# A linear-attention and MoE kernel: output turned by VectorE's block transposes, key transposes parted

## The reference

```python
for t in range(S):                                   # attention with a decaying state
    state = alpha[:, :, t, :, None] * state + einsum('bhd,bhe->bhde', k[:, :, t], v[:, :, t])
    y[:, :, t] = einsum('bhd,bhde->bhe', q[:, :, t], state)
x = y as (3072 tokens, 384)
p = domain_probs / (domain_probs.sum(-1) + 1e-9)     # dense mixture, 4 experts of 1024
x = sum_e p[:, e] * (relu(x @ w1[e]) @ w2[e])
h = x @ w_in                                         # 384 -> 2048
out = (h * clip(h + 3, 0, 6) / 6) @ w_out
```

## Time and profile before

| | |
|---|---|
| median of 3 runs | 1420.34 us (1420.33 to 1421.3) |
| profiled execution | 1419.88 us, its span 1418.1 |
| busy share of the span | TensorE 98%, VectorE 52%, ScalarE 38%, POOL 59% |
| mean granted clock of TensorE | 0.996 |

### The profile page before, as it was taken

One profiled execution on the slowest core, in us unless ns is written; L12 is line 12 of the kernel. 1 busy time (PEld: TensorE's weight loads), 2 busy tenths in 40 slices (PEclk: granted clock), 3 DMA queues, 4 the chain that ended last, 5 costly groups with the idle time before them and its releaser, 6 DMA issues.

```text
span 1418.1 us, 30461 instructions
## 1 busy us (share of the span) xinstructions
PE 1388.5 (98%) x11672; PEld 1140.5 (80%) x11672; DVE 731.3 (52%) x1383; ACT 533.6 (38%) x927; POOL 837.6 (59%) x870
## 2 busy tenths in 40 slices
PE   6789999999999999999999999999999999999998
PEld 5678888888888888888888888888888888888887
DVE  6977665545554555455545455555455343333343
ACT  2133333333344333344433335433334443335553
POOL 8867776565666565656665656565655444444442
PEclk9899999999999999999999999999999999999999
DMA  4333333333333433334333333443332333233330
GB/s 142 119 120 108 102 110 96 106 93 115 93 104 124 138 93 107 93 109 128 107 115 116 93 107 93 136 123 107 93 93 82 113 118 100 90 100 92 99 123 34
DMA packets 70366, 150.10 MB, mean 106 GB/s; under 512 B 9296, under 2 KB 21840, under 8 KB 70224
## 3 DMA queue, kind: packets, MB, share of 16 engines
q1 hardware_dynamic: 70224, 148.16, 34.5%
HBM read 143.36 MB, written 4.77 MB: 104 GB/s over the span
## 4 chain that ended last, share of the span: by engine, by line
PE 93%; POOL 4%; issue 1%; DVE 1%; ACT 0%; DMA 0%; DVEq 0%; POOLq 0%; ACTq 0%
PE h_bank L446 41%; PE out_banks L462 28%; PE out_third L462 14%; PE score_banks L358 4%; POOL k_lev L828 2%; PE score_banks L420 2%; PE turn_bank L398 1%; POOL decay L802 1%; PE score_banks L414 1%; PE turn_bank L386 1%; PE turn_bank L388 1%; POOL w_lo L842 1%; PE turn_bank L374 1%; POOL k_lev L818 0%; DMA alpha_q<-qa 0%
## 5 line engine op out<-in xcount | busy, mean ns | idle before, releaser
L842 POOL TENSOR_TENSOR w_lo<-w_raw,w_hi 128x768 fp32r<-128x768 f32 x288 | 547.6, 1902 | 528.2 <-ACT w_hi L745 528.0
L739 ACT ACTIVATE h_hi<-gated 128x512 fp32r<-128x512 f32 x288 | 182.2, 633 | 670.5 <-DVE gated L590 582.3
L446 PE MATMUL h_bank<-x_hi,w_hi 128*128 128x512 f32 x864 | 336.4, 389 | 1.1 <-issue 1.1
L446 PE MATMUL h_bank<-x_lo,w_hi 128*128 128x512 f32 x864 | 336.1, 389 | 0.0
L446 PE MATMUL h_bank<-x_hi,w_lo 128*128 128x512 f32 x864 | 336.0, 389 | 0.0
L590 DVE SCALAR_TENSOR_TENSOR gated<-h_bank,probs 128x512 f32<-128x512 f32 x192 | 132.7, 691 | 328.0 <-PE h_bank L446 328.0
L604 DVE TENSOR_TENSOR h_lo<-gated,h_hi 128x512 fp32r<-128x512 f32 x288 | 241.6, 839 | 57.5 <-ACT h_hi L739 57.5
L745 ACT ACTIVATE w_hi<-w_raw 128x768 fp32r<-128x768 f32 x288 | 239.1, 830 | 8.0 <-DMA w_raw<-w 8.0
L462 PE MATMUL out_banks<-h_hi,w_hi 128*128 128x512 f32 x576 | 233.0, 405 | 0.3 <-DVE x_lo L614 0.3
L462 PE MATMUL out_banks<-h_hi,w_lo 128*128 128x512 f32 x576 | 225.0, 391 | 0.0
L462 PE MATMUL out_banks<-h_lo,w_hi 128*128 128x512 f32 x576 | 224.5, 390 | 0.0
(11 more groups left out here) (75 smaller groups left out, 1279.5 us busy)
## 6 DMA issues: line engine op xcount, KB each, us to landing
w_raw<-w SPq DMA_DIRECT2D x288, 384.0 KB, 3.1
alpha_q<-qa SPq DMA_DIRECT2D x48, 256.0 KB, 3.5
k_raw<-kk SPq DMA_DIRECT2D x48, 128.0 KB, 3.5
probs<-prob_scratch SPq DMA_DIRECT2D x6, 1024.0 KB, 7.5
v_diag<-v SPq DMA_DIRECT2D x96, 48.0 KB, 2.4
out<-result SPq DMA_DIRECT2D x18, 256.0 KB, 3.9
level_sb<-level SPq DMA_DIRECT2D x1, 80.0 KB, 3.1
ident_sb<-ident SPq DMA_DIRECT2D x1, 64.0 KB, 2.8
```

The source lines that it names most:

```text
L446: mm = pe.matmul(h_bank[g % 2][:, :], a, x, start=k == 0 and i == 0, stop=k == K3 - 1 and i == 2)
L739: act.activation(h_hi[:, g % DEEP, :], gated[:, g % 2, :], ACT.Copy).then_inc(hh_made, 1)
L842: pool.tensor_tensor(w_lo[:, g % RING, :], w_raw[:, g % RAW, :], w_hi[:, g % RING, :].bitcast(F32), ALU.subtract).then_inc(w_lo_made, 1)
```

## The change

- `attend` writes its output in another order. Weights are now 32 tokens wide instead of 64, and each matmul goes to a quarter of the partitions (`quarter(i, jp)`): eight matmuls instead of four, then sixteen instead of eight. Partitions then hold (head of the pair, pair half, 32 tokens), the free dimension (token half, 96 features).
- `copy_y` and TensorE's `turn_y` go. VectorE's new `turn_y` has two block transposes of 32x32, each of 64 partitions and 192 elements, from PSUM to `y_turned`. The rows of the first weights are ordered on the host to fit.
- `split_x` reads `y_turned`, one slot behind the state slot.
- `turn_k(n)` is parted: `turn_k(n, 0)` stays in the score visit, `turn_k(n, 1)` ends the attention visit of chunk n - 1. ScalarE copies each half for itself; the copy of half 1 stands in the slot behind the state slot. Half 0 waits for that copy. `next_state` waits for the transpose that ends its visit.
- `decay_state` moves from VectorE to ScalarE, as four activations of 48 elements, in the slot behind the score slot; in the first stage it stands ahead of `odd_k`.

The core of the diff; left out are renamed semaphores (`ys_made` is now `yt_made`), doubled counts, `TURN_AT`, buffer declarations and the order of the weight rows.

```diff
@@ -204,6 +203,10 @@
         def own(i):
             return slice(64 * i, 64 * i + 64)
+        def quarter(i, jp):
+            return slice(64 * i + 32 * jp, 64 * i + 32 * jp + 32)
         def alpha_of(n):
             return alpha_q[n % QRING][:, 0, :, :]
...
@@ -359,40 +362,22 @@
                                                start=True, stop=True)
                 mm.then_inc(p_made, 1)
-            def turn_k(n):
+            def turn_k(n, jp):
                 if n == 0:
                     pe.wait_ge(in_ident, 16)
                 pe.wait_ge(k_made, K_STEPS * (n + 1))
-                need(pe, s_made, carried(n))
-                need(pe, x_hi_made, n - 1)
-                need(pe, x_lo_made, n - 1)
-                if n % PER_TILE == 0:
-                    need(pe, x_hi_made, n)
-                    need(pe, x_lo_made, n)
-                for jp in range(2):
-                    mm = pe.transpose(kt_out[:, jp * P:(jp + 1) * P], k_level(n, LEVELS)[:, 2 * jp:2 * jp + 2, :],
-                                      ident_sb[:, :])
-                mm.then_inc(kt_made, 1)
-            def turn_y(n):
-                pe.wait_ge(ys_made, 2 * (n + 1))
-                need(pe, s_made, carried(n + 1))
-                need(pe, x_hi_made, n)
-                need(pe, x_lo_made, n)
-                rows = y_rows[n % 2]
-                for i in range(2):
-                    pe.matmul(turn_bank[own(i), P:P + CH], rows[:, P:STATE], ident_sb[:, own(i)],
-                              start=True, stop=True)
-                pe.transpose(turn_bank[:, 0:P], rows[:, 0:P], ident_sb[:, :]).then_inc(xt_made, 1)
+                if jp == 0 or n <= PER_TILE:
+                    need(pe, s_made, carried(n))
+                if jp == 0 and n > PER_TILE:
+                    pe.wait_ge(kn_made, 2 * carried(n) + 1)
+                pe.transpose(kt_out[:, jp * P:(jp + 1) * P], k_level(n, LEVELS)[:, 2 * jp:2 * jp + 2, :],
+                             ident_sb[:, :]).then_inc(kt_made, 1)
             def carry(n):
                 pe.wait_ge(in_v[n % 2], 32 * (n // 2 + 1))
-                pe.wait_ge(kn_made, carried(n) + 1)
-                need(pe, x_hi_made, n)
-                need(pe, x_lo_made, n)
+                pe.wait_ge(kn_made, 2 * (carried(n) + 1))
                 for jp in range(2):
                     for i in range(2):
                         mm = pe.matmul(kv_out[own(i), jp * 2 * HEAD_D:(jp + 1) * 2 * HEAD_D],
...
@@ -408,18 +393,22 @@
                 pe.wait_ge(q_made, Q_STEPS * (n + 1))
                 need(pe, s_made, carried(n))
                 pe.wait_ge(keep_made, KEEPS * (n + 1))
-                for jp in range(2):
-                    for i in range(2):
-                        lo = 512 * i + jp * 2 * HEAD_D
-                        mm = pe.matmul(y_out[own(i), lo:lo + 2 * HEAD_D], p_kept[:, i, jp, :],
-                                       v_diag[n % 2][:, :, jp, i, :], start=jp == 0, stop=not inter,
-                                       skip_group_check=True)
-                for j in range(PAIRS if inter else 0):
-                    for i in range(2):
-                        lo = 512 * i + j * HEAD_D
-                        mm = pe.matmul(y_out[own(i), lo:lo + HEAD_D], q_level(n, LEVELS)[own(i), j, :],
-                                       state[n % 2][own(i), j, :], start=False, stop=True,
-                                       skip_group_check=True)
+                for th in range(2):
+                    for jp in range(2):
+                        for i in range(2):
+                            lo = 512 * i + th * 2 * HEAD_D
+                            mm = pe.matmul(y_out[quarter(i, jp), lo:lo + 2 * HEAD_D],
+                                           p_kept[:, i, jp, 32 * th:32 * th + 32], v_diag[n % 2][:, :, jp, i, :],
+                                           start=th == 0, stop=not inter, skip_group_check=True)
+                for th in range(2 if inter else 0):
+                    for jj in range(2):
+                        for jp in range(2):
+                            for i in range(2):
+                                j, lo = 2 * jp + jj, 512 * i + (2 * th + jj) * HEAD_D
+                                mm = pe.matmul(y_out[quarter(i, jp), lo:lo + HEAD_D],
+                                               q_level(n, LEVELS)[own(i), j, 32 * th:32 * th + 32],
+                                               state[n % 2][own(i), j, :], start=False, stop=True,
+                                               skip_group_check=True)
                 mm.then_inc(y_made, 1)
             def keep_warm(n):
...
@@ -474,25 +464,24 @@
                 carry(n)
                 attend(n)
                 keep_warm(2)
-                turn_y(n)
+                turn_k(n + 1, 1)
                 if n + 1 < PER_TILE:
-                    turn_k(n + 1)
+                    turn_k(n + 1, 0)
                 keep_warm(2)
             for g in range(SLOTS):
                 hidden(g)
                 if g in SCORE_AT:
                     n = SCORE_AT[g]
                     score(n)
-                    if n % PER_TILE > 0:
-                        turn_y(n - 1)
                     if not last_of_seq(n):
-                        turn_k(n)
+                        turn_k(n, 0)
                 if g in STATE_AT:
-                    if not last_of_seq(STATE_AT[g]):
-                        carry(STATE_AT[g])
-                    attend(STATE_AT[g])
-                if g in TURN_AT:
-                    turn_y(TURN_AT[g])
+                    n = STATE_AT[g]
+                    if not last_of_seq(n):
+                        carry(n)
+                    attend(n)
+                    if n + 1 < CHUNKS and not last_of_seq(n + 1):
+                        turn_k(n + 1, 1)
                 if g >= BEHIND:
                     project(g - BEHIND)
             for g in range(SLOTS - BEHIND, SLOTS):
@@ -550,34 +539,35 @@
                                     s[:, :, at:at + CH // 2].rearrange("p a (m x) -> p a m x", x=x)
                                     ).then_inc(keep_made, 1)
-            def decay_state(n):
-                dve.wait_ge(s_made, carried(n))
-                dve.wait_ge(z_made, Z_STEPS * (n + 1))
-                dve.tensor_tensor(state_decayed[:, :, :], state[n % 2][:, :, :],
-                                  total[n % 2][:, :].rearrange("p (j o) -> p j o", o=1
-                                                               ).to_broadcast([P, PAIRS, HEAD_D]),
-                                  ALU.mult).then_inc(dec_made, 1)
             def next_state(n):
                 kv = kv_out.rearrange("p (j e) -> p j e", e=HEAD_D)
                 need(dve, y_made, n)
                 dve.wait_ge(kv_made, carried(n) + 1)
+                if n >= PER_TILE and n + 1 < CHUNKS and not last_of_seq(n + 1):
+                    dve.wait_ge(kt_made, 2 * carried(n + 1) + 1)
                 if first_of_seq(n):
                     op = dve.tensor_copy(state[(n + 1) % 2][:, :, :], kv)
                 else:
-                    dve.wait_ge(dec_made, decayed(n) + 1)
+                    dve.wait_ge(dec_made, PAIRS * (decayed(n) + 1))
                     op = dve.tensor_tensor(state[(n + 1) % 2][:, :, :], state_decayed[:, :, :], kv, ALU.add)
                 op.then_inc(s_made, 1)
+            def turn_y(n):
+                dve.wait_ge(y_made, n + 1)
+                need(dve, x_hi_made, n - 1)
+                need(dve, x_lo_made, n - 1)
+                for i in range(2):
+                    dve.transpose(y_turned[n % 2][own(i), :, :].rearrange("p b (h t) -> p h b t", t=32),
+                                  scores(n)[own(i), 512 * i:512 * i + STATE].rearrange(
+                                      "p (h b e) -> p h b e", h=2, e=32)).then_inc(yt_made, 1)
             def split_x(n):
                 r, cols = x_cols(n)
                 dve.wait_ge(x_hi_made, n + 1)
-                if (n + 1) % PER_TILE and not last_of_seq(n + 1):
-                    dve.wait_ge(kn_made, carried(n + 1) + 1)
-                dve.tensor_tensor(x_lo[:, r, :, cols], kv_out.rearrange("p (k t) -> p k t", t=CH),
+                dve.tensor_tensor(x_lo[:, r, :, cols], y_turned[n % 2][:, :, :],
                                   x_hi[:, r, :, cols].bitcast(F32), ALU.subtract).then_inc(x_lo_made, 1)
             def weigh_hidden(g):
...
@@ -655,9 +645,8 @@
                     split_x(n - 1)
                 for step in range(3):
                     scale_q(n + 2, step)
-                if not first_of_seq(n):
-                    decay_state(n)
                 next_state(n)
+                turn_y(n)
                 for step in range(3, Q_STEPS):
                     scale_q(n + 2, step)
                 if n < 2:
@@ -669,18 +658,16 @@
                     hidden_lo(g - 1)
                 (weigh_hidden if PHASES[PHASE_OF[g]][0] == "E" else gate_hidden)(g)
                 if g - 1 in SCORE_AT:
```

(93 more changed lines are left out.)

6 lines of the change are left out of this document (3 added, 3 removed).

## The result

The changed kernel takes 1431.6 us (1430.4 to 1433.4, 4 runs) where the kernel before takes 1420.8 on the same chip: a ratio of 1.0079 [1.0067, 1.0092]. It is slower; 1413 us, with 1405 to 1421, was forecast. The profiled execution took 1432.3 us, its span 1430.5.

A forecast was written before the change was run, and what follows sets the result against it. TensorE's matrix work, busy 98%, was taken as the bound, with VectorE full in the first stage. 1419.9 - 15.7 + 4.3 + 3.2 + 1.0 = 1412.7, said as 1413 us, range 1405 to 1421.

The forecast's parts named there:

- TensorE's work: Chunks 8 to 47: visits save 19.6 us, added key transposes, shape changes and narrower tiles considered, net -15.7 us.
- The shape change and four narrow tiles at a time: In attend: changing tile shape costs 0.13 us, +4.7 over 36 visits; second part in eight rounds of four, -4.7.
- The two waits: Score visits in slots 3 and 21: TensorE waits for ScalarE's key copy, some 5 and 3 us, adding +4.3 and +3.2.
- its bound of 5.1: Slot 21: +3.2, with +1.9 more if a query step falls behind one more POOL subtraction.
- rival (a): Slot 3: the clock falls behind the 5 us gap, about 9 us at half speed lose 4.5, giving 1417; chance 0.25.
- Nothing for all this: Slots, engines other than TensorE: VectorE's and ScalarE's added work counted as zero; without cover up to 0.3 + 0.7 a chunk.
- VectorE ... some +0.3 a chunk: Slots: VectorE drops the decay and takes two turns out of PSUM, some +0.3 us a chunk in 24 us.
- a `project` and a `hidden` (4.1 us): Slots: room for weigh_hidden, queued with query steps and hidden_lo behind next_state, which waits 1.2 us longer.
- The first 80.7 us. I take +1.0: First stage: waits for y_made and decays ahead of odd_k against shorter chain; +1.0 us, bounds -2.5 and +3.
- (e): VectorE's turn is slow, or its wait for y holds the first stage; at 1.0 us a turn, 1423; chance 0.05.
- two turns of 0.35 replace it, 0: First stage: two VectorE turns of 0.35 us replace its decay of 0.70, no net cost.

The follow-up runs named there:

- experiment 6: Changed kernel with only VectorE's split_x one slot later, the copy of key half 1 left in place: 1422.2 us, 1.0014.
- experiment 5: Changed kernel with the copy of key half 1 at the end of its own state slot and VectorE's split_x one slot later: 1407.7 us, 0.9913.
- Experiments 9 and 12: 9: changed kernel, first-stage turns doubled, 1436.4 us; 12: changed kernel with early key copy, late split, reordered first stage, first-stage decay back on VectorE, 1409.4 us.
- experiment 8: Changed kernel with key copy early and first stage reordered: VectorE's turn behind query steps, ScalarE's split a chunk later, odd_k ahead of decays: 1421.4 us, 1.0004.
- experiment 7: Changed kernel with VectorE's split_x in its place but reading one input, y_turned times a constant: 1427.5 us, 1.0049.
- experiment 1: Changed kernel with ScalarE's copy of key half 1 at the end of its own state slot instead of one slot later: 1424.4 us, 1.0021.

## Why the prediction was wrong, point by point

- **TensorE's work: right.** -15.7 us was forecast. From chunk 16 on a chunk is 0.41 to 0.43 us shorter (28.02 us from one `attend` to the next for 28.45), some 16.4 over forty. The shape change and four narrow tiles at a time came out within 0.03 us a visit of their prices.
- **The two waits: right in place and chain.** In slot 3 it is 5.9 us for 5. From one `attend` to the next, slot 3 costs 6.8 us more than before; without the clock's 2.7 and with the half microsecond that the visit saves, the wait is worth 4.6, for 4.3. Slot 21: 5.6 us for 3, worth 5.5 for 3.2, above its bound of 5.1; experiment 6 gives 1.6 of it to the split, and the query steps have 0.8.
- **The clock: rival (a), at 0.25, came true** in slot 3 and again in slot 21, which it did not name: 2.7 and 1.9 us, and in this trace 2.7 more in slot 0 (1.6 in the matmuls, 1.1 in the score visit). It had 4.5 for slot 3 alone. The clock is not the whole error: without its 7.3 us the profiled execution would take 1425, still outside the range.
- **"Nothing for all this" is the step that failed.** The term "VectorE ... some +0.3 a chunk" left the new split at the price of the old one out of PSUM and gave its wait for ScalarE no time. A chunk has 1.9 us of idle time and 1.1 more of busy time in the split, and 0.8 more in its query steps. The cover named, "a `project` and a `hidden` (4.1 us)", holds for `weigh_hidden` in most slots. It does not hold for `collect` at the four phase changes (0.95 us each, 3.8), nor in three more crowded slots (2.6): at 157 us TensorE waits for masks, at 168 and 188 us for the key copy. All of these go in experiment 5 but 0.3 us. With the key copy early, moving the split out of the masks' way gave 16.7 us; with the copy late, 9.4. That the split moved past ScalarE's `weights_hi`, the very instruction that releases POOL's `w_lo`, was to be read from the diff. By the Trainium skill's rule on the page named above the split would have been given a wait of up to POOL's 1.84 us, an estimate.
- **"The first 80.7 us. I take +1.0" was the other one:** +6.4 measured, outside its bound of +3. The nearest rival is (e), at 0.05, but its price did not come: the turn is 0.38 us, not 0.8. VectorE's busy time in the stretch that ends with the first `hidden` (35.00 to 80.70 before, to 87.05 after) rises from 41.56 to 44.54 us, its idle time from 4.14 to 7.51. VectorE was full; "two turns of 0.35 replace it, 0" was nearly right for the turns (4.6 us from 35 us on, for the decay's 4.2) but left out the dearer split (3.9 for 2.5) and the wait for y. Experiments 9 and 12 show that what is added to VectorE's program comes out by three quarters or more; experiment 8 shows that the wait for y alone is not the price, since the turn put later holds TensorE instead, and experiment 7 that the dearer split alone is not.

Beyond 1412.7 us the terms give: first stage 5.4; slot 3 0.3 and slot 21 2.3; clock 7.3; phase changes 3.8; three small waits 2.6; visits -0.7. That is 21.0, for the 19.6 of the profiled execution. What stays open is the first stage: its 6.4 us are 4.3 to 6.4 in traces of the same program, and they are not shared out between VectorE's work, its idle time and the clock. The clock is a rival that no run tested there: its granted mean from 35 us to the first `hidden` is 0.80, where it was 0.89 before.

## What to carry to other kernels

When an instruction is moved, or its operand goes from PSUM to SBUF, price it by what will run beside it: a VectorE instruction with two SBUF inputs, released by the same engine that releases a GpSimd one, met it in all 40 chunks of the slots here. Making that one instruction short is not enough (4.1 us in experiment 7), since the next one meets it instead; the place in the queue has to change. A pair of halves made by two engines goes wrong where the second half stands directly behind the first one's wait; a slot of distance gave 16.7 us here with the key copy early, and 9.4 with it late. And an engine at half its time can still be the one in whose queue the critical instructions stand: look at what is queued behind each new wait, not at shares.

## What the hardware showed that was not expected

- A 128x192 subtraction took 0.35 us with one operand in PSUM, 1.68 with both in SBUF beside POOL's 1.84 us subtraction, and 0.35 (the median of experiment 5) with both in SBUF a slot later. An instruction with one SBUF input took 0.35 in the first place, beside POOL.
- Float32 tiles of 128 rows and 32 columns run four together: four rounds of 96 moving columns in about 0.33 us (16 records, 0.46 with the shape change).
- With 32 weight columns instead of 64 a round of four records took 44 ns, (243.65 - 243.17 - 0.13) / 8, for 58: 11 ns a record, below the 16 that could be read as a floor. Two records are one float32 matmul, so that is 22 ns a matmul.
- A TensorE wait of 5.9 us was followed by 5 us of matmuls at the lower clock level. Of two waits for masks in experiment 1, the one of 2.4 us at 112 us was followed by matmuls at full speed, the one of 2.5 at 151 us by matmuls 0.43 us apart until 155.
